# A prologue with a bank and a buffer for each of its three groups, and fifteen unused identity matmuls on TensorE

## The reference

```python
for c in range(nc):                       # chunks of 32 queries
    k_full = concat([mem_k, k[:, :, max(0, 32*c - 16): min(S, 32*c + 40)]])   # 8 + up to 56 keys
    v_full = ...                          # the same window of v
    a = softmax(q_c @ k_full.T / 8)
    out[:, :, chunk] = a @ v_full
x = out as (3072, 512)
x = max(x @ w1, x @ w2, x @ w3) @ w_out            # 512 -> 768 -> 512
h = x @ w_in                                        # 512 -> 2048
g = 0 if h <= -1, h if h >= 1, (h + 1)**2 / 4 between
result = g @ w_out2                                 # 2048 -> 512
```

## Time and profile before

| | |
|---|---|
| median of three executions | 987.39 us (986.23 to 987.53) |
| the profiled execution, its own time | 987.29 us |
| its span, first to last instruction | 985.4 us |
| TensorE busy | 969.7 us, 98% of the span |
| VectorE, ScalarE, GpSimd busy | 48%, 36%, 15% |
| granted clock as printed | 1.00 |

### The profile page before, as it was taken

One profiled execution on the slowest core, in us unless ns is written; L12 is line 12 of the kernel. 1 busy time (PEld: TensorE's weight loads), 2 busy tenths in 40 slices (PEclk: granted clock), 3 DMA queues, 4 the chain that ended last, 5 costly groups with the idle time before them and its releaser, 6 DMA issues.

```text
span 985.4 us, 18546 instructions
## 1 busy us (share of the span) xinstructions
PE 969.7 (98%) x7968; PEld 905.5 (92%) x7968; DVE 470.4 (48%) x713; ACT 354.4 (36%) x553; POOL 150.1 (15%) x176
## 2 busy tenths in 40 slices
PE   5999999999999999999999999999999999999998
PEld 4999999999999999999988988899888898888897
DVE  4572514334242433425456655566545666454452
ACT  3341222222122222222344535544354544444253
POOL 1103352315225231000000000000000000000000
PEclk9999999999999999999999999999999999999999
DMA  9453643635555461042736566655656545574532
GB/s 372 174 196 106 247 184 138 252 123 194 183 214 177 178 230 61 1 171 65 259 130 206 205 236 209 208 192 200 248 185 243 192 160 195 188 258 172 192 118 107
DMA packets 32206, 181.52 MB, mean 184 GB/s; under 512 B 3456, under 2 KB 7552, under 8 KB 21888
## 3 DMA queue, kind: packets, MB, share of 16 engines
q0 software_dynamic: 9216, 92.28, 26.8%
q1 hardware_dynamic: 22912, 88.09, 24.3%
HBM read 144.70 MB, written 35.65 MB: 183 GB/s over the span
## 4 chain that ended last, share of the span: by engine, by line
PE 98%; DVE 1%; ACT 1%; DMA 0%; issue 0%
PE mlp L465 23%; PE mlp L466 23%; PE mlp L467 23%; PE attn_ps L467 3%; PE attn_ps L466 3%; PE attn_ps L465 3%; PE scores_ps L467 3%; PE scores_ps L466 3%; PE scores_ps L465 3%; PE attn_ps L458 3%; PE scores_ps L434 2%; PE trans_ps L467 1%; PE trans_ps L466 1%; PE trans_ps L465 1%; PE trans_ps L441 1%; DMA qk_raw<-qk_l 0%
## 5 line engine op out<-in xcount | busy, mean ns | idle before, releaser
L465 PE MATMUL mlp<-x_hi,w_hi 128*128 128x384 f32 x576 | 197.5, 343 | 1.6 <-issue 1.6
L467 PE MATMUL mlp<-x_lo,w_hi 128*128 128x384 f32 x576 | 193.6, 336 | 0.0
L466 PE MATMUL mlp<-x_hi,w_lo 128*128 128x384 f32 x576 | 193.3, 336 | 0.0
L466 PE MATMUL mlp<-yc,wi 128*128 128x384 f32 x448 | 150.7, 336 | 0.0
L467 PE MATMUL mlp<-yc,wi 128*128 128x384 f32 x448 | 149.6, 334 | 0.0
L465 PE MATMUL mlp<-yc,wi 128*128 128x384 f32 x448 | 149.6, 334 | 0.0
L747 ACT ACTIVATE ramp<-up,half_col 128x768 f32<-128x768 f32 x64 | 60.1, 939 | 197.4 <-DVE up L961 178.3
L465 PEld LDWEIGHTS mlp<-x_hi,w_hi 128*128 128x128 f32 x576 | 108.8, 189 | 3.7 <-issue 1.9
L466 PEld LDWEIGHTS mlp<-x_hi,w_lo 128*128 128x128 f32 x576 | 108.9, 189 | 0.0
L467 PEld LDWEIGHTS mlp<-x_lo,w_hi 128*128 128x128 f32 x576 | 108.7, 189 | 0.0
L466 PEld LDWEIGHTS mlp<-yc,wi 128*128 128x128 f32 x448 | 84.1, 188 | 8.8
(11 more groups left out here) (111 smaller groups left out, 1644.8 us busy)
## 6 DMA issues: line engine op xcount, KB each, us to landing
wi<-wi_scratch POOLq DMA_DIRECT2D x32, 1792.0 KB, 7.6
wo<-wo_scratch POOLq DMA_DIRECT2D x32, 1024.0 KB, 5.1
qk_raw<-qk_l SPq DMA_DIRECT2D x24, 768.0 KB, 8.2
wi_scratch<-stage_a SPq DMA_DIRECT2D x8, 1792.0 KB, 8.0
v_raw<-v_l SPq DMA_DIRECT2D x24, 512.0 KB, 4.8
wo_scratch<-stage_a SPq DMA_DIRECT2D x8, 1024.0 KB, 6.6
y_scratch<-y_stage SPq DMA_DIRECT2D x32, 192.0 KB, 2.5
y_raw<-y_scratch SPq DMA_DIRECT2D x8, 768.0 KB, 5.4
```

The source lines that it names most:

```text
L465: pe.matmul(out_ap, a_hi, b_hi, start=first, stop=False, skip_group_check=beside)
L466: pe.matmul(out_ap, a_lo, b_hi, start=False, stop=False, skip_group_check=beside)
L467: return pe.matmul(out_ap, a_hi, b_lo, start=False, stop=last, skip_group_check=beside)
```

## The change

It changes the prologue only, with the shared buffers that it uses.

1. Banks: the three `mlp` banks become one tensor, `mlp_ps`. The scores of groups 0, 1, 2 go to `scores_ps`, `mlp_ps` and `attn_ps`. Their shifted scores go to three parts of `y_stage`, which nothing else uses yet. Their exponentials go to the two banks of `scores_ps` and to `mlp[2]`. The weighted sums of group 1 go to `mlp_ps`. The transposes of group 2 go to `mlp[2]` and their copy to `score`.
2. Waits: scores 1 and 2 no longer wait for a shift, and weighted sums and transposes only for what their new banks need. VectorE's shift waits for the shift before it.
3. Loads: the first five are qk 0, qk 1, qk 2, v 0, weight piece 0; and v 3 comes ahead of weight piece 2.
4. Orders: on ScalarE `w_high(0)` goes ahead of transposed 0, and exponential 2 ahead of x_high 0; on VectorE shift 1 goes ahead of scale 0 and shift 2 ahead of scale 1, and the three x_low come last; on TensorE transposes 2 go ahead of weighted_v 1.
5. The first `layer1` group runs its eight matmuls with `x_hi` before it waits for the last `x_lo`, then the four with `x_lo`.
6. `keep_busy` issues 5, 1, 3, 2, 2 and 2 matmuls of the identity with itself (128x128, full precision) between the steps on TensorE. Each writes a bank that the next real matmul there writes anew.

```diff
-        mlp = [psum(f"mlp{i}", BANK)[:, :] for i in range(3)]
+        mlp_ps = psum("mlp_ps", 3 * BANK)
+        mlp = [mlp_ps[:, i * BANK:(i + 1) * BANK] for i in range(3)]
...
+        def scores_of(n):
+            ps = (scores_ps, mlp_ps, attn_ps)[n if isinstance(n, int) and n < GPT else 0]
...
+        def score_of(n):
+            if isinstance(n, int) and n < GPT:
+                return y_stage[:, :, :].rearrange("p d t -> p (d t)")[:, n * H * WIN:(n + 1) * H * WIN].rearrange("p (h k) -> p h k", h=H)
+            return score[:, :, :]
...
+        first_e = [x.rearrange("p (h k) -> p h k", h=H) for x in (scores_ps[:, 0:BANK], scores_ps[:, BANK:2 * BANK], mlp[2])]
...
-            load_qk(0)
-            load_qk(1)
+            for j in range(GPT):
+                load_qk(j)
+            load_v(0)
             load_wa(0)
-            load_qk(2)
-            for j in range(GPT):
-                load_v(j)
+            load_v(1)
+            load_v(2)
             load_wa(1)
             load_qk(3)
+            load_v(3)
             load_wa(2)
-            load_v(3)
             load_wa(3)
...
-                if not isinstance(n, int) or n:
+                if not isinstance(n, int) or n >= GPT:
                     pe.wait_ge(sub_done, n)
...
+                if isinstance(t, int) and t == 0 and f == 0 and w == 0:
+                    pe.wait_ge(x_hi_done, GPT)
+                    pe.wait_ge(x_lo_done, GPT - 1)
+                    for k in range(KD):
+                        pe.matmul(bank[:, 0:TT], w123_hi[:, 0, k], x_hi[a][:, k], start=k == 0, stop=False)
+                        pe.matmul(bank[:, 0:TT], w123_lo[:, 0, k], x_hi[a][:, k], start=False, stop=False)
+                    pe.wait_ge(x_lo_done, GPT)
+                    for k in range(KD):
+                        last = pe.matmul(bank[:, 0:TT], w123_hi[:, 0, k], x_lo[a][:, k], start=False, stop=k == KD - 1)
...
+            def keep_busy(count, bank):
+                for _ in range(count):
+                    pe.matmul(bank[:, 0:P], ident[:, :], ident[:, :], start=True, stop=True)
+            keep_busy(5, trans_ps[:, :])
             scores_ready(0, 0, 0)
-            scores(0)
+            scores(0, 0)
+            keep_busy(1, trans_ps[:, :])
             scores_ready(1, 1, 0)
-            scores(1)
+            scores(1, 1)
+            keep_busy(3, trans_ps[:, :])
+            scores_ready(2, 2, 0)
+            scores(2, 2)
+            keep_busy(2, trans_ps[:, :])
             transposes(0, 0)
-            scores_ready(2, 2, 0)
-            scores(2)
             weights_ready(0, 0, 0)
-            weighted_v(0)
+            pe.wait_ge(sub_done, GPT)
+            keep_busy(2, attn_ps[:, :])
+            weighted_v(0, 0)
             transposes(1, 1)
+            transposes(2, 0)
             weights_ready(1, 1, 0)
-            weighted_v(1)
-            transposes(2, 0)
+            weighted_v(1, 1)
             weights_ready(2, 2, 0)
-            weighted_v(2)
+            pe.wait_ge(x_lo_done, 1)
+            weighted_v(2, 2)
+            keep_busy(2, scores_ps[:, :])
             tile_a(0, 0, True, True)
...
             first_exponent(0)
-            transposed(0)
             first_exponent(1)
             w_high(0)
+            transposed(0)
+            first_exponent(2)
             x_high(0, 0, 0)
-            first_exponent(2)
             transposed(1)
+            transposed(2)
             x_high(1, 0, 1)
-            transposed(2)
             x_high(2, 0, 2)
             w_high(1)
...
             softmax_shift(0, 0, 0)
+            softmax_shift(1, 1, 0)
             softmax_scale(0, 0, first_e[0])
-            softmax_shift(1, 1, 0)
+            softmax_shift(2, 2, 0)
             softmax_scale(1, 1, first_e[1])
-            softmax_shift(2, 2, 0)
-            x_low(0, 0, 0)
             softmax_scale(2, 0, first_e[2])
-            x_low(1, 0, 1)
-            x_low(2, 0, 2)
+            for j in range(GPT):
+                x_low(j, 0, j)
```

More of the change, by code:

```diff
@@ L433, in scores @@
                             rows = slice(r * D, (r + 1) * D)
-                            last = pe.matmul(scores_v[part, r, i], q[rows, i, part], k[rows, i, c], start=True, stop=True)
+                            last = pe.matmul(s[part, r, i], q[rows, i, part], k[rows, i, c], start=True, stop=True)
                 last.then_inc(scores_done, 1)
@@ L439, in transposes @@
                 pe.wait_ge(prob_done, n + 1)
+                if isinstance(n, int) and n == 1:
+                    pe.wait_ge(prob_t_done, 1)
                 for m in range(HALF_HEADS):
-                    last = pe.transpose(trans_v[:, m], prob[:, slot, 2 * m:2 * m + 2], ident[:, :])
+                    last = pe.transpose(trans_of(n)[:, m * P:(m + 1) * P], prob[:, slot, 2 * m:2 * m + 2], ident[:, :])
                 last.then_inc(trans_done, 1)
@@ L447, in weights_ready, with weighted_v @@
                 pe.wait_ge(prob_t_done, n + 1)
-                if not isinstance(n, int) or n:
+                if not isinstance(n, int) or n >= GPT:
                     pe.wait_ge(x_lo_done, n)
-            def weighted_v(j):
+            def weighted_v(n, j):
+                o = sums_of(n).rearrange("p i (m c q) -> p i m c q", m=2, c=CPG)
                 for m in range(2):
@@ L457, in weighted_v @@
                                 rows = slice(i * D, (i + 1) * D)
-                                last = pe.matmul(attn_o[r * D:(r + 1) * D, i, m, c], v_raw[rows, j, 2 * m + r, c],
-                                                 prob_t[rows, 2 * m + r, c], start=True, stop=True)
+                                last = pe.matmul(o[r * D:(r + 1) * D, i, m, c], v_raw[rows, j, 2 * m + r, c],
+                                                 prob_t_of(n)[rows, 2 * m + r, c], start=True, stop=True)
                 last.then_inc(attn_done, 1)
@@ L516, in tile_a @@
                     if attention and r == 0 and j:
-                        weighted_v(j - 1)
-                        scores(j)
-                    if f == 0:
+                        weighted_v(n0 + j - 1, j - 1)
+                        scores(n0 + j, j)
+                    if f == 0 and not first:
                         pe.wait_ge(x_lo_done, GPT * (t + 1))
@@ L522, in tile_a @@
                     if attention and f == 0:
-                        scores(0)
+                        scores(n0, 0)
                     if attention and r:
@@ L528, in tile_a @@
                 if attention:
-                    weighted_v(GPT - 1)
+                    weighted_v(n0 + GPT - 1, GPT - 1)
                 if t < TILES - 1:
@@ L828, in x_low @@
                 dve.wait_ge(x_hi_done, n + 1)
-                dve.tensor_tensor(x_of(x_lo[x], j), attn_x, x_of(x_hi[x], j).bitcast(F32), ALU.subtract).then_inc(x_lo_done, 1)
+                dve.tensor_tensor(x_of(x_lo[x], j), sums_x(n), x_of(x_hi[x], j).bitcast(F32), ALU.subtract).then_inc(x_lo_done, 1)
             def w_low(n):
```

52 lines of the change are left out of this document (30 added, 22 removed).

## The result

The changed kernel takes 984.89 us (median of 14, 983.89 to 985.91) against 986.6 (median of 14, 986.21 to 987.53): ratio 0.998, interval 0.9973 to 0.9987. It is faster by 1.7 us; the forecast was 6.8.

A forecast was written before the change was run, and what follows sets the result against it. TensorE bounds the kernel, busy 98% of the span, its clock low through the prologue; an earlier layer1 start and clock rise move the mark from 30.18 to 23.4 us, so 987.29 - 6.8 = 980.5 us, range 979.3 to 986.3.

The forecast's parts named there:

- the mark: First matmul of the second layer1 bank, layer1(0, 0, 0, 1), at 30.18 us before; forecast at 23.4.
- three signs that the prediction named for a wrong forecast: Clock falling between 12 and 16 us, identity matmuls above 0.64 us, or a weight piece landing after 12.5 us.
- the sum, with the high clock from before 14 us: TensorE's prologue at the high clock: first layer1 matmul at 20.35 us, 6.8 us gained, 980.5 us.
- the hold: TensorE's clock, risen early in the scores and identity matmuls, stays high through the prologue; chance 0.53, 979.5 to 982 us.
- the identity pair: Two identity matmuls on TensorE before weighted_v(0), from 14.3 to 14.75 us; 0.44 us high clock, 1.12 low.
- the second rival: Clock low until layer1, never risen or risen and fallen near 13 us; 986.6 us (984.4 to 987.3), chance 0.22.
- the first (a rise in the sums): Rival: clock rises between 14 and 24 us; the mark at 25.75, gain 4.4 us, 982.9 us, chance 0.21.
- The transposes rule of the Trainium skill: Transposes on TensorE do not count as busy in the same way, so the clock would be gone again; no size.
- the weight piece's landing: Weight piece 0, now the fifth load, lands at about 12.1 us; a late piece, 992.0 us, had chance 0.04.
- ScalarE's queue as the dear part: w_high(0) waits for its weight piece, 12.1 to 13.6 us; weighted_v(0) starts no earlier than 14.3, against 13.3.
- The first group's split: First layer1 group runs eight matmuls before the last x_lo; saves about 0.75 us before the first matmul.
- The end of the argument: Prologue's last part: transposes 2 from 16.75 us, weighted_v 1 and 2 to 19.5, first layer1 matmul 20.35, the mark 23.4.

The follow-up runs named there:

- e2: The changed kernel with twelve more identity matmuls behind the first transposes; 984.79 us, ratio 0.9986 to the kernel before.
- e15: The changed kernel with weight piece 0's copy later, qk 3 and weight piece 1 held until the first weighted sum, loads from v 3 until the third; 980.32 us.
- e17: The changed kernel with only the two holds of the loads from e15, weight copy as in the change; 983.58 us, ratio 0.9965.
- e3: The changed kernel with ScalarE's copy of weight piece 0 behind the first transposed copy and the third exponential; 983.6 us, ratio 0.9971.
- e1: The changed kernel without its fifteen identity matmuls; 983.68 us, ratio 0.9973 to the kernel before.
- e10: The changed kernel without identity matmuls once more, on the same chip as a repeat of the changed kernel; 984.0 us, ratio 0.9972.
- e4: The kernel before with fifteen identity matmuls added and its own banks, loads and orders; 988.38 us, ratio 1.0015.
- e6: The changed kernel with e3's later copy, and weight piece 1 and all loads behind it held until the first weighted sum; 981.98 us, ratio 0.9951.
- e7: e6 without identity matmuls, on the same chip; 984.51 us, ratio 0.9974.
- e16: e15 without its identity matmuls, on a different chip; 984.03 us, ratio 0.9972.
- e8: The changed kernel with each identity matmul written as one 16-bit matmul of 512 columns, one record and not two; 984.68 us, ratio 0.9979.
- e11: The changed kernel itself again, on the chip of e10; 985.3 us, ratio 0.9986.
- e12: The kernel before with only the first layer1 group changed, eight x_hi matmuls ahead of the wait for the last x_lo; 986.31 us against 986.74.
- e9: The changed kernel with e3's later copy and qk 3, now ahead of weight piece 1, held with the loads behind until the first weighted sum; 982.02 us.

## Why the prediction was wrong

**Direction and place were right, the size was not.** The gain lies ahead of the mark and nothing behind it waits. The time is inside the range, but far from 980.5. Two of the three signs that the prediction named for a wrong forecast came: a clock that fell between 12 and 16 us (14.08) and a weight piece that landed after 12.5 (12.92).

**The step that failed first is "the sum, with the high clock from before 14 us".** The rise came as I argued, at 10.67. It did not hold: the clock fell at 14.08, inside the gap that I had worked out myself (12.3 to 14.3, in truth 12.15 to 15.00). I gave the hold 0.53 with no row for it. Against the forecast, in the profiled execution: the identity pair 1.19 us and not 0.45, weighted_v 0 1.87 and not 1.06, transposes to weighted_v 1 0.4 more, weighted_v 1 and 2 0.3 more. That is 2.25 of the 4.2 us between my mark (23.4) and the measured one (27.57). What ran was the second rival up to 20.9 (risen and fallen) and then the first (a rise in the sums), and its time lies between theirs. The transposes rule of the Trainium skill (TensorE: Matmul & The Clock Gate, section Part 4: PE-mode transpose), which I set beside it, is neither shown nor refuted: in e2 and e15 they ran between other work and the clock held, and in the change they were followed by a gap.

**A term was missing: the supply of instructions.** I priced the identity matmuls by their time on TensorE alone. They are also 30 records, a quarter of a block. The rows for this term were in the trace of before: the 0.40 us of "issue" in the middle of the first weighted sum, behind 221 records, at 14.18. The prediction has no word on it. In the change it cost 0.93 us ahead of the mark; first matmul and the rest of scores(3) make 0.3 more.

**A size was off: the weight piece's landing.** I put it at 12.1, it landed at 12.92, 9.92 us after its issue. The bytes ahead of it were the ones that I had counted, but it landed 2.8 us behind v 0 (2.12 + 8.0 = 10.1), where 768 KB took 1.9 us in the rows of before. An instruction packet ran from 10.50 to 11.51 in between; whether it held the piece up was not tested. The pair began at 15.0 and not 14.3: 0.7 us. With 2.25, 1.2 and 0.7 the 4.2 us are told.

**Right:** the chain on VectorE (shift 2 ending at 12.75, forecast 13.0), ScalarE's queue as the dear part, 1.12 us for the pair at the low clock (1.19). For a row of them 0.56 was too much: ten records came in 2.47 us, 0.213 from start to start, which makes 0.43 for one, the figure that the prediction set beside its own; at the high clock it is 0.22, as put. The best end of the second rival was added up wrongly as well: with the rise before layer1 its mark is 24.8 + 12 x 0.173 + 0.95 = 27.8 and its time 984.9, not 984.4. The first group's split was worth 0.6 us of the start, about as put.

**The end of the argument held when its two premises were made true.** e15, with a gap under 1.2 us and the loads out of the way of the instruction blocks, has its mark at 23.12 and takes 980.3. It is not the forecast's kernel: its pair begins at 12.99 and not at 14.3. But in both TensorE then waits for the third group's `prob` (to 16.42, forecast 16.75), and from there to the mark the forecast had 6.6 us and e15 took 6.7. e17 shows that holding the loads alone did not do it, e3 that the order alone did not. What the identity matmuls are worth depends on that: nothing or a loss in the change (e1, e10), a loss in the old order (e4), 2.5 us in e6 against e7 and 4 in e15 against e16.

The granted clocks of all executions fit this. With the gap of 2.8 us and more (the change, e8, e11, e17) the clock is at most 0.998 in all 41 executions, so it fell in each; with none over 1.1 us and no stall (e15) it is 0.999 or more in all five.

**Open.** Why the kernel without them raises its clock at 18 to 21 us in some executions and at 28 in others was not tried. How much of the 1.7 us comes from banks and how much from orders was not separated; e12 puts the layer1 split at 0.4 by its medians, with an interval from a loss of 0.3 to a gain of 1.5. The two cures in the change's own order together, the gap filled as in e2 and the loads held, were not run; e15 takes the gap away by another order, which also moves the first weighted sum 2.5 us ahead.

## What to carry to other kernels

Work put into an engine's gap only to keep its clock pays if no gap is left in which the clock falls, so look for the longest remaining gap before counting what the clock gives. Matmuls cost instructions as well as time: where a chain says "issue" between two matmuls that have no wait between them, count the records up to it, and compare the counts over several versions. Early loads that nobody needs yet can hold back what the engine needs to run at all; holding them cost nothing in e15, where each still landed before its use, and 2.2 us in e6's profiled execution, where qk 3 did not.

## What the runs showed of the hardware that was not expected

- TensorE stood 0.40 to 2.33 us in the middle of uninterrupted groups of matmuls, always behind 221 or 222, 349 or 475 records, until 1.3 to 1.6 us after an instruction packet of 16 KB had landed. In the 2 us before, the DMA engines moved 368 to 420 GB/s (204 before one of e2's).
- The granted clock fell at 14.08, 14.41, 15.89 and 13.65 in the four profiles with a gap of 2.8 to 3.0 us on TensorE before 15.1 (the change, e8, e11, e17), and behind stalls of 1.76 (e3) and 1.53 us (e9). It held through gaps of 1.1 us (e15), through 1.40 in e2 and through 2.33 in e11, so between 1.5 and 2.4 us the length of a gap alone did not decide.
- Without identity matmuls executions of one kernel differed by 3.5 us (983.16 to 986.63), and four profiles go with where the clock rose: 982.82 and 982.97 us with 18.39 and 20.57, 985.96 and 985.78 with 28.17 and 28.11.
